# Strips of one weight group and back products of the group before it take turns, and the work behind a strip is spread over later chunks

## The chip, the cores and the metric

The kernel runs on one core of a Trainium2 chip. The metric is the device time of one execution in microseconds (us). Of the core's engines, TensorE (PE) does the matmuls, VectorE (DVE) and ScalarE (ACT) do the elementwise work that reads and writes the matmul accumulators (PSUM), GpSimd (POOL) prepares the weights, and SyncE (SP) issues the DMAs. Each engine works through its own list of instructions in order. They wait for one another through semaphores.

## The reference

Windowed attention with sinks for 2 batches x 8 heads x 768 positions x 64, then two feed-forward layers on the 1536 tokens (512 wide):

```python
keep = is_sink | in_window            # 4 sinks, window 128
a = softmax(where(keep, scale * q @ k.T, -1e9))
x = (a @ v) as 1536 x 512
# layer B, 1536 hidden columns
g = x @ w_gate
x = (g * sigmoid(g) * (x @ w_val)) @ w_out
# layer C, 2048 hidden columns
h = x @ w_in
out = (max(h, 0) + alpha * min(h, 0)) @ w_out2
```

## The kernel before

Every matmul operand is kept as a rounded part and the rest (`_hi`, `_lo`), and a product is three matmuls: hi x hi, hi x lo, lo x hi. A weight group g is 256 hidden columns: layer B has groups 0 to 5, of which group 5 comes first in what follows, layer C has groups 0 to 7. The tokens are three blocks of 512: block 0 ("single") is computed plainly, blocks 1 and 2 ("the pair") together, by a Strassen-like scheme.

The list `plan` sets the order of everything. Its entries for PE are chunks:

- a **front** (line 1881): a hidden tile of block 0, in two halves of 6 matmuls;
- a **strip** (line 1940): 6 matmuls, one of the 7 products (numbers 0 to 6) that together make one *set*, that is the four hidden tiles h11, h12, h21, h22 of the pair (first digit: half of the group, second: block 1 or 2). Layer B has two sets for a group, the gates set (in the banks of `att_ps`) and the values set (one bank of `att_ps`, two of `ffn_ps`), layer C one set;
- a **back product** (line 1966), here also "back": 6 matmuls, hidden tiles times output weights. A pair group has 8: four for block 1, which read h11 and h21, then four for block 2, which read h12 and h22.

What follows a strip: ACT copies strip 0 aside (`keep`, line 2098). DVE adds strips together in five `mix` steps 0 to 4, behind strips 1, 3, 4, 5, 6 (lines 2232, 2235, 2238, 2241, 2244). Strip 2 waits for `keep`, strips 3, 5 and 6 wait for mixes 0, 1 and 2. In layer B, ACT makes `silu` of the gates (line 2066). In layer C it makes `relu`, two instructions a tile (lines 2085, 2087). Then every hidden tile goes through three steps: **product** on DVE (2283 in B, 2294 in C), **rounding** on ACT (2108), **rest** on DVE (2300). In the plan, `("hidden", h)` stands for product and rounding, `("rest", h)` for the rest. The first of the back products of a block waits for the rests of both hidden tiles that it reads. A strip that starts in a bank waits until the tile that stood there is used up: the first strip in a bank of a layer C set waits for the rest of the tile of the set ahead, h11 for strip 0, h21 for strip 1, h12 for strip 4. Behind every back DVE takes the result out of PSUM (`evac`, 2309, 2325).

`emit(chunk, now, *later)` (line 888) writes the chunk, the events `now`, then what earlier chunks left for this place, and leaves `later[0]` for the next chunk, `later[1]` for the one behind it. Before the change layer B runs, group by group, 7 gates strips of group g+1, 8 backs of group g, 7 values strips of group g+1. Layer C runs 7 strips of group g+1, then 8 backs of group g. POOL prepares the weights in its own order (`jobs`), far ahead.

## Time and profile before

| | |
|---|---|
| median of 3 runs | 639.23 us (639.03 to 640.42) |
| the profiled execution | 640.56 us, its span 638.8 us |
| PE busy | 622.8 us, 97% of the span |
| DVE, ACT, POOL busy | 410.1, 244.3, 451.8 us (64%, 38%, 71%) |
| chain that ended last | PE 85%, DVE 7%, ACT 3%, issue 3% |
| granted clock of PE in every slice | 9 tenths or more |

To read it: a matmul instruction of 512 columns is shown as busy for about 0.39 us but the next one starts about 0.23 us later, so they overlap, and a busy PE can still start chunks late. What counts is the distance between the starts of chunks.

The strips begin at 227 us with those of layer B group 5. Layer B's pair runs until 421 us, with fronts between. Layer C's strips begin at 443 us, and its last matmul starts at 635 us.

### The profile page before, as it was taken

What the parts mean: (1) busy time and instruction counts of PE and PEld (TensorE: products, weight loads), DVE (VectorE), ACT (ScalarE), POOL (GpSimd) and SP (SyncE); (2) the same over time, 40 slices, a digit from 0 to 9 for tenths busy, and PEclk for the clock granted to TensorE, in tenths of its full rate; (3) what the DMA queues carried; (4) which work ended last, traced back from release to release, by engine and by line L of the source; (5) the groups of instructions that cost most, each with busy time, mean ns of one, the idle gap of its engine ahead of it and who ended that gap; (6) DMA issues with size and microseconds to landing.
All of it is one profiled execution on the core that took longest, in us unless ns stands there. A gap on an engine that the chain in (4) does not pass through costs nothing.

```text
span 638.8 us, 9474 instructions
## 1 busy us (share of the span) xinstructions
PE 622.8 (97%) x3072; PEld 488.0 (76%) x3072; DVE 410.1 (64%) x696; ACT 244.3 (38%) x585; POOL 451.8 (71%) x600
## 2 busy tenths in 40 slices
PE   8889999999999999999999999999999999999998
PEld 5467676776776888878788878888788888888886
DVE  4954566655476876564656474799686567756474
ACT  4735644545534642121212121435544333442150
POOL 6848698796985889998989664779999887810000
PEclk9999999999999999999999999999999999999999
DMA  9343323311331011221202222000212222000004
GB/s 299 110 149 110 123 80 136 117 51 50 100 95 43 30 35 34 76 74 48 67 33 67 82 84 63 25 30 16 67 67 66 67 66 84 17 0 1 1 14 184
DMA packets 29391, 45.67 MB, mean 71 GB/s; under 512 B 2880, under 2 KB 9024, under 8 KB 29344
## 3 DMA queue, kind: packets, MB, share of 16 engines
q1 hardware_dynamic: 29200, 44.81, 21.7%
q8 instruction: 25, 0.41, 0.3%
q10 hardware_dynamic: 144, 0.26, 0.1%
q14 instruction: 22, 0.18, 0.1%
HBM read 41.92 MB, written 3.15 MB: 71 GB/s over the span
## 4 chain that ended last, share of the span: by engine, by line
PE 85%; DVE 7%; ACT 3%; issue 3%; DMA 1%; POOL 0%; SPq 0%; DVEq 0%; ACTq 0%; POOLq 0%
PE ffn_ps L1966 27%; PE att_ps L1940 22%; PE ffn_ps L1881 14%; PE att_ps L1966 7%; PE ffn_ps L1940 6%; PE att_ps L1830 3%; PE att_ps L1792 2%; PE att_ps L1809 1%; DVE scratch L2193 1%; ACT scratch L2008 1%; PE att_ps L1881 1%; DVE scratch L2309 1%; ACT L2008 1%; DMA raw_weights<-pieces 1%; PE ffn_ps L1830 1%
## 5 line engine op out<-in xcount | busy, mean ns | idle before, releaser
L1653 POOL TENSOR_TENSOR w_lo<-raw_weights,w_hi 128x512 fp32r<-128x512 f32 (+1 forms) x128 | 154.4, 1206 | 10.3
L1652 POOL CAST w_hi<-raw_weights 128x512 fp32r<-128x512 f32 (+1 forms) x128 | 79.2, 619 | 38.0 <-PE ffn_ps L1966 20.5
L2309 DVE TENSOR_TENSOR scratch<-ffn_ps,scratch 128x512 f32<-128x512 f32 x112 | 76.4, 687 | 34.9 <-PE ffn_ps L1966 34.2
L1681 POOL TENSOR_TENSOR w_lo<-part_sum,w_hi 128x256 fp32r<-128x256 f32 x80 | 61.1, 764 | 6.4
L1881 PE MATMUL ffn_ps<-x_hi,w_hi 128*128 128x512 f32 x152 | 61.8, 406 | 2.1 <-DVE x_lo L2330 1.0
L1881 PE MATMUL ffn_ps<-x_hi,w_lo 128*128 128x512 f32 x152 | 59.5, 391 | 0.0
L1881 PE MATMUL ffn_ps<-x_lo,w_hi 128*128 128x512 f32 x152 | 59.2, 390 | 0.0
L1733 POOL TENSOR_TENSOR scratch<-scratch,inv 128x264 f32<-128x264 f32 (+1 forms) x48 | 31.2, 649 | 31.8 <-DVE inv L2182 31.5
L1966 PE MATMUL ffn_ps<-h_hi,w_hi 128*128 128x512 f32 x130 | 51.6, 397 | 0.0
L1966 PE MATMUL ffn_ps<-h_hi,w_lo 128*128 128x512 f32 x130 | 50.7, 390 | 0.0
L1966 PE MATMUL ffn_ps<-h_lo,w_hi 128*128 128x512 f32 x130 | 50.6, 389 | 0.0
L2098 ACT ACTIVATE value_sb<-att_ps 128x512 f32<-128x512 f32 x14 | 8.4, 600 | 100.3 <-PE att_ps L1940 100.3
L1940 PE MATMUL att_ps<-t_hi,w_hi 128*128 128x512 f32 x112 | 44.5, 398 | 1.3 <-DVE gate_sb L2232 0.8
L1940 PE MATMUL att_ps<-t_hi,w_lo 128*128 128x512 f32 x112 | 44.0, 392 | 0.0
L1940 PE MATMUL att_ps<-t_lo,w_hi 128*128 128x512 f32 x112 | 43.7, 391 | 0.0
L1940 PE MATMUL att_ps<-x_hi,w_hi 128*128 128x512 f32 x108 | 42.7, 395 | 0.0
L1940 PE MATMUL att_ps<-x_hi,w_lo 128*128 128x512 f32 x108 | 42.5, 393 | 0.0
L1940 PE MATMUL att_ps<-x_lo,w_hi 128*128 128x512 f32 x108 | 42.1, 390 | 0.0
L2003 ACT ACTIVATE bias<-top 128x2 f32<-128x2 f32 x48 | 9.8, 203 | 75.5 <-DVE top L2177 75.0
L1680 POOL CAST w_hi<-part_sum 128x256 fp32r<-128x256 f32 x80 | 34.7, 434 | 5.1
L2166 DVE COPY_PREDICATED att_ps<-take_prev,att_ps 128x256 f32<-128x256 int32 x34 | 14.4, 425 | 35.8 <-PE att_ps L1792 22.3
L2087 ACT ACTIVATE gate_sb<-gate_sb,minus_alpha 128x512 f32<-128x512 f32 x48 | 34.8, 725 | 1.6
(207 smaller groups left out, 1574.9 us busy)
## 6 DMA issues: line engine op xcount, KB each, us to landing
raw_weights<-pieces SPq DMA_DIRECT2D x122, 256.0 KB, 2.7
k_sb<-kt SPq DMA_DIRECT2D x12, 264.0 KB, 3.4
v_sb<-vt SPq DMA_DIRECT2D x12, 256.0 KB, 2.7
out<-scratch SPq DMA_DIRECT2D x12, 256.0 KB, 2.0
q_sb<-qt SPq DMA_DIRECT2D x11, 256.0 KB, 3.5
scratch<-vs SPq DMA_DIRECT2D x1, 384.0 KB, 5.5
q_sb<-qt ACTq DMA_DIRECT2D x1, 256.0 KB, 2.8
alpha<-alpha_t SPq DMA_DIRECT2D x1, 8.0 KB, 6.6
```

The source lines that it names most:

```text
L1652: chain(pool.tensor_copy(hi, raw[:, r % n_raw, at]))
L1653: last = pool.tensor_tensor(lo, raw[:, r % n_raw, at], hi.bitcast(F32), ALU.subtract)
L1680: chain(pool.tensor_copy(hi, s))
L1681: pool.tensor_tensor(lo, s, hi.bitcast(F32), ALU.subtract).then_inc(split_done, 1)
L1733: pool.tensor_tensor(rows, rows, inv[:, u % 4, :].unsqueeze(2).to_broadcast([P, 2, cols - at]), ALU.mult).then_inc(norm_done, 1)
L1830: last = pe.matmul(x[d, g, :], v_sb[:, ring, g, d], pt_sb[:, u % 2, m, h, :], start=g == 0 and m == 0, stop=not has_prev(c), skip_group_ch ...
L1881: last = pe.matmul(ps, w_parts[a][:, block_cols(kk)], x_parts(kk)[b], start=kk == 0 and (a, b) == (0, 0), stop=kk == n_k - 1 and (a, b) == ...
L1940: last = pe.matmul(ps, w_parts[a][:, block_cols(at * half_k + kk)], b_parts[b][:, kk, :], start=first and kk == 0 and (a, b) == (0, 0), st ...
L1966: last = pe.matmul(ps, lhs, rhs, start=f == 0 and (a, b) == (0, 0), stop=f == F - 1 and (a, b) == (1, 0))
L2087: act.activation(gate_of(h), gate_of(h), ACT.Copy, scale=minus_alpha[:, col:col + 1]).then_inc(relu_done, 1)
L2166: last = dve.copy_predicated(own_keys, take_prev[:, :].bitcast(mybir.dt.int32).unsqueeze(1).to_broadcast([P, 2, P]), s[:, :, 0:P])
L2309: ins = dve.tensor_tensor(total, back_ps(key), total, ALU.add)
```

## The change

The chunks stand in another order, by a new helper `weave`. In layer B the gates strips of group g+1 are put between the backs of group g for block 1: strips 0, 1, 2, back, 3, back, 4, back, 5, back, 6. The values strips are put between the backs for block 2: 0, back, 1, back, 2, back, 3, back, 4, 5, 6. For the first pair group (5) the gates strips take turns with the backs of layer C group 2, and its values strips stand alone. In layer C strips and backs alternate one by one: 0, back, 1, back, ..., 6, back, back. The first two sets of C are exceptions: group 0 runs 0, back, 1, 2, 3, back, 4, back, 5, 6, back, group 1 runs 0, 1, back, 2, back, ...

The events behind a strip move too. The backs of layer B for the pair use two banks of `ffn_ps` in turn, where they used five, and a wait of the values strips for an evac falls away. No instruction is added or dropped.

```diff
+    def weave(first, second, ahead):
+        order, left = [], list(first)
+        for n, chunk in zip(ahead, second):
+            order += left[:n] + [chunk]
+            left = left[n:]
+        return order + left
...
             elif g[0] == "B":
-                now = {2: [("hidden", h11)], 3: [mixes[1]], 4: [mixes[2], ("rest", h11), ("hidden", h22)],
-                       5: [mixes[3], ("hidden", h21)], 6: [mixes[4], ("rest", h22)]}[i]
-                emit(chunk, now, *([[("hidden", h12)], [("rest", h21)], [("rest", h12)]] if i == 6 else []))
+                now, later = {2: ([("hidden", h11)], [[], [], [("rest", h11)]]), 3: ([mixes[1]], []),
+                              4: ([mixes[2]], [[("hidden", h22)]]), 5: ([mixes[3]], [[("hidden", h21)]]),
+                              6: ([mixes[4]], [[("rest", h22), ("hidden", h12)], [("rest", h21)], [("rest", h12)]])}[i]
+                emit(chunk, now, *later)
             else:
-                now = {2: [("relu", h11)], 3: [mixes[1]], 4: [mixes[2], ("relu", h22), ("hidden", h11)],
-                       5: [mixes[3], ("relu", h21), ("rest", h11)], 6: [mixes[4], ("relu", h12), ("hidden", h22)]}[i]
-                emit(chunk, now, *([[("hidden", h21)], [("rest", h22)], [("hidden", h12)], [("rest", h21)], [("rest", h12)]]
-                                   if i == 6 else []))
+                now = {2: [], 3: [mixes[1]], 4: [mixes[2]], 5: [mixes[3]], 6: [mixes[4]]}[i]
+                done = {2: h11, 4: h22, 5: h21, 6: h12}.get(i)
+                if done:
+                    emit(chunk, now + [("relu", done)], [], [("hidden", done)], [("rest", done)])
+                else:
+                    emit(chunk, now)
...
-    fill = fronts(groups_c[1]) + backs(groups_c[0]) + fronts(groups_c[2]) + backs(groups_c[1]) + strips(pair_b[0], 0)
+    fill = (fronts(groups_c[1]) + backs(groups_c[0]) + fronts(groups_c[2]) + backs(groups_c[1])
+            + weave(strips(pair_b[0], 0), backs(groups_c[2]), (2, 1, 1, 1)))
...
+    plan_b = strips(pair_b[0], 1)
+    for g, ahead in zip(pair_b, pair_b[1:]):
+        in_gates, in_values = ([("back", (g, t, d)) for d in range(4)] for t in pair)
+        plan_b += weave(strips(ahead, 0), in_gates, (3, 1, 1, 1)) + weave(strips(ahead, 1), in_values, (1, 1, 1, 1))
...
-    turn = (backs(groups_c[3]) + fronts(groups_c[4]) + fronts(groups_c[5]) + backs(groups_c[4]) + strips(groups_c[0], 0))
+    turn = (backs(groups_c[3]) + fronts(groups_c[4]) + fronts(groups_c[5]) + backs(groups_c[4])
+            + weave(strips(groups_c[0], 0), backs(groups_c[5]), (1, 3, 1, 2)))
...
+    for g, ahead in zip(groups_c, groups_c[1:]):
+        plan_c += weave(strips(ahead, 0), pair_backs(g), (2 if g == groups_c[0] else 1,) + 6 * (1,) + (0,))
...
-                home = (rest_of_b if g != pair_b[-1] else (2, 3, 4, 0, 1, 2, 3, 4))[4 * (t - 1) + d]
+                home = d % 2 if g != pair_b[-1] else (2, 3, 4, 0, 1, 2, 3, 4)[4 * (t - 1) + d]
...
-                    if kind == "V":
-                        pe.wait_ge(evac_done, max(n for key, n in back_no.items() if back_home[key] == 2 + role and n < back_no[m[0], 1, 0]))
```

The order on DVE where a values set of layer B ends and the next gates set begins (lines 2232 to 2244 are the mixes, 2283 products, 2300 rests), before:

```order
L2300 TENSOR_TENSOR h_lo<-att_ps,h_hi 128x512
L2283 TENSOR_TENSOR value_sb<-value_sb,gate_sb 128x512
L2241 TENSOR_TENSOR ffn_ps<-ffn_ps,value_sb 128x512
L2283 TENSOR_TENSOR ffn_ps<-ffn_ps,gate_sb 128x512
L2244 TENSOR_TENSOR ffn_ps<-ffn_ps,value_sb 128x512
L2300 TENSOR_TENSOR h_lo<-value_sb,h_hi 128x512
L2283 TENSOR_TENSOR ffn_ps<-ffn_ps,gate_sb 128x512
L2232 TENSOR_TENSOR gate_sb<-att_ps,gate_sb 128x512
L2300 TENSOR_TENSOR h_lo<-ffn_ps,h_hi 128x512 x2
L2235 TENSOR_TENSOR gate_sb<-att_ps,gate_sb 128x512
```

The same place on DVE in the changed kernel, whose lines are numbered 4 higher:

```order
L2304 TENSOR_TENSOR h_lo<-att_ps,h_hi 128x512
L2242 TENSOR_TENSOR value_sb<-ffn_ps,value_sb 128x512
L2245 TENSOR_TENSOR ffn_ps<-ffn_ps,value_sb 128x512
L2287 TENSOR_TENSOR value_sb<-value_sb,gate_sb 128x512
L2248 TENSOR_TENSOR ffn_ps<-ffn_ps,value_sb 128x512
L2287 TENSOR_TENSOR ffn_ps<-ffn_ps,gate_sb 128x512
L2304 TENSOR_TENSOR h_lo<-value_sb,h_hi 128x512
L2287 TENSOR_TENSOR ffn_ps<-ffn_ps,gate_sb 128x512
L2236 TENSOR_TENSOR gate_sb<-att_ps,gate_sb 128x512
L2304 TENSOR_TENSOR h_lo<-ffn_ps,h_hi 128x512 x2
L2313 TENSOR_TENSOR scratch<-ffn_ps,scratch 128x512
```

The rest of h11 and the products of h22 and h21 changed places with mixes 2 to 4. From the rest of h22 on, the order is the old one, except that evacs now follow at once: the first back stands three strips behind the set, where it stood seven.

The order on DVE where the set of layer C group 0 ends and that of group 1 begins (2241, 2244 mixes 3 and 4, 2294 products, 2309 evacs), before:

```order
L2244 TENSOR_TENSOR att_ps<-att_ps,value_sb 128x512
L2294 SCALAR_TENSOR_TENSOR value_sb<-value_sb,gate_sb 128x512
L2309 TENSOR_TENSOR scratch<-att_ps,scratch 128x512
L2294 SCALAR_TENSOR_TENSOR att_ps<-att_ps,gate_sb 128x512
L2309 TENSOR_TENSOR scratch<-ffn_ps,scratch 128x512
L2300 TENSOR_TENSOR h_lo<-value_sb,h_hi 128x512
L2309 TENSOR_TENSOR scratch<-ffn_ps,scratch 128x512
L2294 SCALAR_TENSOR_TENSOR att_ps<-att_ps,gate_sb 128x512
L2309 TENSOR_TENSOR scratch<-att_ps,scratch 128x512
L2300 TENSOR_TENSOR w_lo<-att_ps,w_hi 128x512 x2
L2232 TENSOR_TENSOR value_sb<-att_ps,value_sb 128x512
```

The same place on DVE in the changed kernel:

```order
L2245 TENSOR_TENSOR att_ps<-att_ps,value_sb 128x512
L2298 SCALAR_TENSOR_TENSOR value_sb<-value_sb,gate_sb 128x512
L2248 TENSOR_TENSOR att_ps<-att_ps,value_sb 128x512
L2304 TENSOR_TENSOR h_lo<-value_sb,h_hi 128x512
L2313 TENSOR_TENSOR scratch<-att_ps,scratch 128x512
L2298 SCALAR_TENSOR_TENSOR att_ps<-att_ps,gate_sb 128x512
L2304 TENSOR_TENSOR w_lo<-att_ps,w_hi 128x512
L2298 SCALAR_TENSOR_TENSOR att_ps<-att_ps,gate_sb 128x512
L2236 TENSOR_TENSOR value_sb<-att_ps,value_sb 128x512
L2304 TENSOR_TENSOR w_lo<-att_ps,w_hi 128x512
```

Four evacs stood between mix 4 and the rest of h21. One is left, since only one back now stands between strip 6 of group 0 and strip 0 of group 1; and the rest of h22 now stands ahead of the product of h21.

## Rows read from the trace of the kernel before

**Rows 1.** Waits of PE, 227 to 640 us: us in total, times, longest.

```profile
PE att_ps L1940 <- DVE gate_sb L2232: 0.8, 2, 0.6
PE att_ps L1940 <- DVE w_lo L2300: 0.4, 1, 0.4
```

**Rows 2.** Chain of waits: start us, us, what, matmuls.

```profile
475.54 1.36 PE att_ps L1966 x6
...
479.62 9.66 PE att_ps L1940 x42
489.28 1.38 PE att_ps L1966 x6
```

**Rows 3.** Timeline of PE, last strips: start us, us, instruction, idle before and releaser.

```profile
312.60 0.40 PE L1940 MATMUL att_ps<-x_hi,w_hi 128*128 128x512 f32 x1
...
317.48 0.47 PE L1940 MATMUL att_ps<-t_hi,w_hi 128*128 128x512 f32 x1 [0.56 <-DVE gate_sb L2232]
317.79 0.40 PE L1940 MATMUL att_ps<-t_lo,w_hi 128*128 128x512 f32 x1
...
318.94 0.39 PE L1940 MATMUL att_ps<-t_hi,w_hi 128*128 128x512 f32 x1
```

**Rows 4.** Timeline of DVE, the same stretch.

```profile
311.24 1.02 DVE L2283 TENSOR_TENSOR value_sb<-value_sb,gate_sb 128x512 f32<-128x512 f32 x1
312.19 0.69 DVE L2241 TENSOR_TENSOR ffn_ps<-ffn_ps,value_sb 128x512 f32<-128x512 f32 x1
312.97 0.70 DVE L2283 TENSOR_TENSOR ffn_ps<-ffn_ps,gate_sb 128x512 f32<-128x512 f32 x1
313.58 0.69 DVE L2244 TENSOR_TENSOR ffn_ps<-ffn_ps,value_sb 128x512 f32<-128x512 f32 x1
314.18 1.72 DVE L2300 TENSOR_TENSOR h_lo<-value_sb,h_hi 128x512 fp32r<-128x512 f32 x1
315.82 0.69 DVE L2283 TENSOR_TENSOR ffn_ps<-ffn_ps,gate_sb 128x512 f32<-128x512 f32 x1
316.64 0.69 DVE L2232 TENSOR_TENSOR gate_sb<-att_ps,gate_sb 128x512 f32<-128x512 f32 x1
317.25 1.28 DVE L2300 TENSOR_TENSOR h_lo<-ffn_ps,h_hi 128x512 fp32r<-128x512 f32 x2
319.14 0.69 DVE L2235 TENSOR_TENSOR gate_sb<-att_ps,gate_sb 128x512 f32<-128x512 f32 x1 [0.61 <-PE att_ps L1940]
```

**Rows 5.** Timeline of PE at another start of a gates set.

```profile
343.64 0.40 PE L1940 MATMUL att_ps<-x_hi,w_hi 128*128 128x512 f32 x1
```

**Rows 6.** Timeline of DVE there.

```profile
347.54 0.68 DVE L2300 TENSOR_TENSOR h_lo<-ffn_ps,h_hi 128x512 fp32r<-128x512 f32 x1
```

**Rows 7.** DVE instructions on value_sb, 240 to 405 us: ns min/median/max.

```profile
L2283 DVE TENSOR_TENSOR value_sb<-value_sb,gate_sb x6: 680/1032/1422, 250.4 to 403.3; 128x512 f32<-128x512 f32 x6
...
L2300 DVE TENSOR_TENSOR h_lo<-value_sb,h_hi x5: 683/1028/1720, 253.0 to 375.9; 128x512 fp32r<-128x512 f32 x5
```

**Rows 8.** Timeline of ACT, the stretch of rows 4.

```profile
313.71 0.60 ACT L2108 ACTIVATE h_hi<-ffn_ps 128x512 fp32r<-128x512 f32 x1 [0.78 <-DVE ffn_ps L2283]
314.20 0.59 ACT L2098 ACTIVATE gate_sb<-att_ps 128x512 f32<-128x512 f32 x1
```

**Rows 9.** Timeline of PE, one strip of stage C.

```profile
460.19 0.47 PE L1940 MATMUL att_ps<-t_hi,w_hi 128*128 128x512 f32 x1 [0.39 <-DVE w_lo L2300]
```

**Rows 10.** Timeline of DVE, stage C.

```profile
530.39 0.69 DVE L2300 TENSOR_TENSOR w_lo<-att_ps,w_hi 128x512 fp32r<-128x512 f32 x1 [0.64 <-ACT w_hi L2108]
531.00 0.69 DVE L2244 TENSOR_TENSOR att_ps<-att_ps,value_sb 128x512 f32<-128x512 f32 x1
```

**Rows 11.** Timeline of ACT, the same stretch.

```profile
529.78 0.58 ACT L2108 ACTIVATE w_hi<-att_ps 128x512 fp32r<-128x512 f32 x1
...
531.80 0.60 ACT L2085 ACTIVATE gate_sb<-att_ps 128x512 f32<-128x512 f32 x1 [0.20 <-DVE att_ps L2244]
...
533.06 0.62 ACT L2108 ACTIVATE w_hi<-value_sb 128x512 fp32r<-128x512 f32 x1
```

More of the change, by code:

```diff
@@ L1010, in parts_of_sums @@
         return [(stage, name, kk) for name in T_PARTS for kk in range(half_k)]
-    fill = fronts(groups_c[1]) + backs(groups_c[0]) + fronts(groups_c[2]) + backs(groups_c[1]) + strips(pair_b[0], 0)
+    fill = (fronts(groups_c[1]) + backs(groups_c[0]) + fronts(groups_c[2]) + backs(groups_c[1])
+            + weave(strips(pair_b[0], 0), backs(groups_c[2]), (2, 1, 1, 1)))
     steps = parts_of_sums("B")
-    low_after = dict(zip((6, 8, 9, 10, 11, 14, 16, 18), steps))
+    low_after = dict(zip((6, 8, 9, 10, 11, 14, 16, 19), steps))
     high_after = dict(zip((5, 7, 8, 9, 10, 13, 15, 17), steps))
@@ L1022, in build_windowed @@
             plan.append(("thi", high_after[n]))
-    for n, g in enumerate(pair_b):
-        if n == 0:
-            for chunk in backs(groups_c[2]) + strips(g, 1):
-                emit_chunk(chunk)
-        if n + 1 < len(pair_b):
-            for chunk in strips(pair_b[n + 1], 0) + pair_backs(g) + strips(pair_b[n + 1], 1):
-                emit_chunk(chunk)
+    plan_b = strips(pair_b[0], 1)
+    for g, ahead in zip(pair_b, pair_b[1:]):
+        in_gates, in_values = ([("back", (g, t, d)) for d in range(4)] for t in pair)
+        plan_b += weave(strips(ahead, 0), in_gates, (3, 1, 1, 1)) + weave(strips(ahead, 1), in_values, (1, 1, 1, 1))
+    for chunk in plan_b:
+        emit_chunk(chunk)
     for chunk in fronts(groups_c[3]):
@@ L1054, in build_windowed @@
             plan.append(("thi", high_after[n]))
-    waiting = backs(groups_c[5])
-    for g in groups_c:
-        if g != groups_c[0]:
-            for chunk in strips(g, 0):
-                emit_chunk(chunk)
-        for chunk in waiting:
-            emit_chunk(chunk)
-        waiting = pair_backs(g)
+    plan_c = []
+    for g, ahead in zip(groups_c, groups_c[1:]):
+        plan_c += weave(strips(ahead, 0), pair_backs(g), (2 if g == groups_c[0] else 1,) + 6 * (1,) + (0,))
         if g[1] >= n_alone:
-            for chunk in fronts(g) + waiting:
-                emit_chunk(chunk)
-            waiting = backs(g)
-    for chunk in waiting:
+            plan_c += backs(g)
+        if ahead[1] >= n_alone:
+            plan_c += fronts(ahead)
+    for chunk in plan_c + pair_backs(groups_c[-1]) + backs(groups_c[-1]):
         emit_chunk(chunk)
@@ L1099, in build_windowed @@
     back_home, front_home, bank_ahead, had = {}, {}, {}, {}
-    rest_of_b = (2, 3, 4, 0, 1, 4, 0, 1)
     in_turn = (3, 4, 0, 1)
```

## The prediction

> **What bounds the kernel now.** I read the waits of the tensor engine first. From the first strip on, PE lost 0.8 us in two waits on a mix and 0.4 us in one wait on a rest [rows 1]. The chain of waits is one row of strips and back products after another: a back takes 1.36 us, seven strips 9.66 us, so 1.38 each, and the first back behind strips 1.38 [rows 2]. So the kernel is bound by the pace at which PE starts matmuls, and a new order can win only what PE still loses at waits. Read by starts, a wait is a little larger than the idle time shown. Take the start of a gates set of layer B, T = 312.60. Strip 3 should start 3 x 1.385 = 4.16 us later and starts at 317.48, 0.72 late. The matmul behind it follows after 0.31 us instead of 0.23, which adds 0.09 [rows 3]. Four gates sets have such a place, this is the largest, and all four come to about 1.9 us. Layer C has one, 0.39 us idle, about 0.5 by starts [rows 9]. More than 2.4 us of waits is not there to be won.
>
> The reason for 317.48 is DVE's list. Mix 0, on which strip 3 waits, stands behind the rest of h22 and the product of h12 and ends at 317.33. Strip 3 starts 0.15 later [rows 3, 4].
>
> **What the change removes.** In the gates sets a back now stands between strips 2 and 3, so strip 3 comes 1.36 us later, more than its lateness of 0.72. In the values sets and the other sets no strip waited before, and the same mixes now have a back of 1.36 us more. So the 1.9 us of layer B go. The dropped evac wait of the values strips showed no time: 0. The two banks for layer B's backs: evacs are done 0.9 us after a back's end (0.20 until DVE starts, as 318.94 to 319.14, and 0.69 [rows 3, 4]), and a bank now comes again two chunks later, 1.36 us at the least, so 0. If the evac were queued behind two more DVE operations, it would show. POOL's order of work is the old one but for two output pieces of layer C, and PE never waited for POOL in these stages [rows 1], so nothing there.
>
> **What it adds in layer B.** The first back of block 1 waits for the rest of h21. It stood seven strips behind T and now stands three behind it, at T + 4.15. When is that rest there? Before: the rest of h22 starts at T + 1.58, the product of h12 at T + 3.22, mix 0 at T + 4.04, the rest of h21 at T + 4.65. It takes 0.68 [rows 6], and PE follows 0.15 later: T + 5.48 [rows 3, 4]. In the new order these four stand in the same sequence. What stands ahead of them is turned round: mix 3 can start 0.20 after its strip, T - 1.18; then the product of h22 at T - 0.58, 0.95 to the next (311.24 to 312.19), mix 4 at T + 0.37, the product of h21 at T + 0.97, the rest of h22 at T + 1.57, with 0.60 for each step. That is the old 1.58. So the rows of before give the new times as they are: the back starts 5.48 - 4.15 = 1.33 us late at this place. At the best one, T = 343.64, the rest of h21 starts at 347.54, T + 3.90, and the lateness is 3.90 + 0.83 - 4.15 = 0.58 [rows 5, 6]. The two others lie between. I take the middle, 0.95, for four places. They differ by how long DVE needs for the two operations on value_sb, 0.68 to 1.72 us [rows 7]. At the fifth place, between groups 5 and 0, both are short (0.68), but the rest of h11 comes in behind mix 3 there, because no backs stand between the values strips: mix 3 at T - 1.18, then six steps of 0.60 up to the product of h12 at T + 2.4, mix 0 0.82 later (as 315.82 to 316.64), the rest of h21 0.61 later at T + 3.85, the back at 4.68: 0.5 late. With 0.09 behind each stop: 4 x 0.95 + 0.5 + 5 x 0.09 = 4.8 us. Bounds: with all operations at 0.68 the rest of h21 is bound by strip 1 (its end T + 2.77, mix 0 at 2.97, rest at 3.58, back at 4.41), 0.25 late at five places, 1.3 us; with 1.33 at each, 7.1 us. ACT lies in the same place: the product of h21 now ends at T + 1.67, was 1.07. Its rounding stands ahead of `keep` (313.71 and 314.20 before, T + 1.11 and 1.60 [rows 8]); `keep` shifts to about T + 2.2 and ends at T + 2.8, when strip 2 is to start (2.77). Some 0.1 us, and inside the lateness of the back, which is counted from T.
>
> On the two operations with value_sb: they took 680 ns at the least, 1.03 us in the median and up to 1.72 [rows 7], and the same instructions with one input in PSUM took 0.68 to 0.70 throughout [rows 4]. The Trainium skill, "SBUF — State Buffer", section "Who interferes with whom", says that a `tensor_tensor` with both inputs in SBUF contends with GpSimd for the shared port and that the loser blocks until the other has finished. By that rule the place of each stop would hang on where GpSimd happens to be, and a set could cost anything between the bounds above; by the rows as they fell, 0.95. The sum takes the rows.
>
> **What it adds in layer C.** First the place between groups 0 and 1. Strip 1 of group 1 starts in the bank of h21 of group 0 and waits for its rest. Between strip 5 of group 0, which completes h21, and this strip stand strip 6, one back and strip 0; there were strip 6, four backs and strip 0. Count from E, the end of strip 5. Mix 3 starts at E + 0.20. From a mix's start, `relu` begins 0.80 later, and the next ACT operation behind its two instructions 2.06 later (531.00, 531.80, 533.06) [rows 10, 11]. So the rounding of h22 is at E + 2.26 and ends at 2.88, its rest at 2.91, the evac of the back at 3.5, the product of h21 at 4.1, ready at 4.8, its rounding until 5.45, its rest 0.03 later (529.78 + 0.58 to 530.39) [rows 10, 11] until 6.2, PE at 6.3. Strip 1 would start at E + 1.38 + 1.36 + 1.38 = 4.1. It is 2.2 us late, 2.3 with the echo. Bounds: 1.5 (if evac and rest of h22 cost nothing) and 3.2 (if an operation on value_sb takes 1.7).
>
> Then the steady sets, groups 1 to 5, each followed by the first back of its block 1. From E: rest of h22 at 2.91, mix 4 behind it at 3.5 (though its strip ends at 2.74), `relu` of h12 from 4.3, and only behind that the rounding of h21, 3.5 + 2.06 = 5.6 to 6.2, its rest 6.2 to 6.9, PE at 7.0. The back stands five chunks behind E, 6.8. Late by 0.2 at five places: 1.0 us. Bounds: 0, and 0.7 each (3.5) where the rest of h22 takes 1.0 more. Before, these rests had four to seven chunks more, and no wait.
>
> **The pace.** Chunks behind a strip take 1.38 to 1.39, others 1.36 [rows 2]. The number of chunks that follow a strip is the same in any order, but more of them are now backs: -0.3 us. Bounds 0 and -2.5 (every strip at 1.36).
>
> **The sum.** -1.9 + 4.8 - 0.5 + 2.3 + 1.0 - 0.3 = +5.4 us. On the profiled execution, 640.56 us (span 638.8 and 1.8 around it), that is 646.0. The median of the runs is 639.23, 1.3 lower, so I forecast 644.5 for it. What a measurement of this kernel tells from no change is 0.2%, 1.3 us.
>
> **Rivals.** (1) *Faster.* The rests are there in time, because DVE, relieved of the crowd behind strips 4 to 6, is earlier than I count. Then the old waits go and no new one comes: -1.9 - 0.5 - 0.3, 636.5 us. It decides at one point: the rest of h21 would have to end by T + 4.0 instead of 4.6 to 5.3, and strip 1 of layer C's group 1 to find its rest 2.2 us earlier. For it: DVE is idle for a third of the time. Against it: mix 0 can't start before strip 1 has ended, so even the lower bound is 0.25 late. (2) *The waits come out at their lower bounds* in layer B (1.3) and in the steady sets (0), and only the place between groups 0 and 1 stands: -1.9 + 1.3 - 0.5 + 2.3 - 0.3 = +0.9, 640.1 us. For it: the operations on value_sb are short when GpSimd is idle, and the steady sets' 0.2 is the difference of two long sums. Against: GpSimd works through most of both layers. (3) *The pace wins more.* Every strip behind a back runs at 1.36: about -2 instead of -0.3, 642.8 us. For it: the first strip behind backs does. Against: the first back behind strips runs at 1.38, so the slow chunk may only have moved. (4) *Worse*: value_sb's operations long at each place, and the steady sets late by 0.5: 4.8 becomes 6.5 and 1.0 becomes 2.5, 647.7 us.
>
> **How the numbers follow.** The forecast 0.50, (1) 0.08, (2) 0.14, (3) 0.13, (4) 0.15. The range 640.4 to 647.4 leaves out (1), part of (2) and half of (4). Faster by over 0.2%: (1) and a tail of (2), 0.10. Within 0.2%, 638.0 to 640.5: half of (2) and little else, 0.10. Slower: 0.80.
>
> **What would show it.** In the profile after: PE idle before the first back of block 1 behind strip 2 of a gates set, with the rest (line 2304) as releaser, 0.5 to 1.3 us at five places; about 2 us before strip 1 of layer C's group 1, near 460 us, with the same releaser; small stops on the same kind of back in layer C's later sets; and no more wait of strip 3 on mix 0. If the first of these is missing, my count of DVE's list is wrong. If strips and backs that alternate all keep 1.36, the pace term is.

## The result, and the profile after

| | before | after |
|---|---|---|
| median | 639.62 us (639.03 to 640.42, 4 runs) | 651.39 us (650.87 to 651.84, 4 runs) |
| ratio | 1 | 1.0184, 95% interval 1.0171 to 1.0196 |
| profiled execution, its span | 640.56, 638.8 us | 651.24, 649.5 us |
| start of the first strip to start of the last matmul | 408.2 us | 418.7 us |

The change costs 11.8 us between the medians and 10.7 us between the two profiled executions. Both profiles start their strips at 227 us, so 10.5 us of it lie between there and the last matmul. The waits of PE from the first strip on, in the changed kernel (total, times, longest; before: [rows 1]):

```profile
PE ffn_ps L1970 <- DVE h_lo L2304: 2.6, 5, 0.6
PE att_ps L1944 <- DVE w_lo L2304: 2.4, 1, 2.4
PE ffn_ps L1970 <- DVE w_lo L2304: 1.1, 1, 1.1
PE att_ps L1970 <- issue: 0.3, 1, 0.3
PE att_ps L1944 <- ACT gate_sb L2102: 0.2, 1, 0.2
```

The waits of strip 3 on mix 0 are gone. Five first backs wait for a rest in layer B (line 1970), one strip waits 2.4 us in layer C, and one first back waits 1.1 us there. That is 6.6 us of idle time against 1.2 before, 5.4 of the 10.5 us.

A wait's idle time is not the whole price, because an engine that is late by less than 0.1 to 0.3 us shows no idle row. So I took the start of every chunk in both traces and subtracted 1.36 us for each, the fastest that a chunk ever ran ([rows 2] has it for backs):

| excess over 1.36 us per chunk | before | after |
|---|---|---|
| stops in layer B, with the chunk behind | 1.9 | 5.8 |
| stop between groups 0 and 1 of layer C, with the chunk behind | 0.65 | 2.7 |
| stops in layer C's steady sets | 0 | 2.7 |
| stops at fronts and at the turn to layer C | 0.35 | 0.6 |
| slow chunks without a stop | 3.0 | 4.6 |
| sum | 5.9 | 16.4 |

A stop is a chunk that starts late because PE waited.

The chain of waits in the changed kernel at the boundary between two groups, with T = 346.32 as the start of strip 0 of the next gates set (start us, us, what):

```profile
342.34 2.77 PE ffn_ps L1944 x12
345.13 0.04 DVE ffn_ps L2245
...
345.74 0.82 DVE value_sb L2287
...
346.86 0.69 DVE ffn_ps L2248
347.55 0.13 DVE ffn_ps L2287
...
348.06 1.27 DVE h_lo L2304
349.33 0.62 DVE ffn_ps L2287
...
350.07 0.57 DVE gate_sb L2236
...
350.68 0.69 DVE h_lo L2304
351.37 0.24 issue
351.62 1.62 PE ffn_ps L1970 x6
353.24 1.39 PE att_ps L1944 x6
354.63 1.39 PE ffn_ps L1970 x6
```

From 345.13 to 351.37 no PE row is in the chain. The end of the kernel hangs on DVE's list: mix 3, product of h22, mix 4, product of h21, rest of h22, product of h12, mix 0, rest of h21. PE's first back starts at 351.62, T + 5.30. With no wait it would start at T + 4.15, the place that the prediction counted for it. Two DVE instructions stand out, the product of h22 (1.20 us) and the rest of h22 (1.27 us). Both have only SBUF inputs. Beside them stand GpSimd's rows:

```profile
344.41 0.61 POOL L1658 CAST w_hi<-raw_weights 128x512 fp32r<-128x512 f32 x1
345.10 1.29 POOL L1659 TENSOR_TENSOR w_lo<-raw_weights,w_hi 128x512 fp32r<-128x512 f32 x1
346.33 1.07 POOL L1658 CAST w_hi<-raw_weights 128x512 fp32r<-128x512 f32 x1
347.49 1.29 POOL L1659 TENSOR_TENSOR w_lo<-raw_weights,w_hi 128x512 fp32r<-128x512 f32 x1
348.72 0.86 POOL L1658 CAST w_hi<-raw_weights 128x256 fp32r<-128x256 f32 x1
```

DVE's product is issued at 345.74. GpSimd's subtraction ends at 346.39, and the product 0.55 later. DVE's rest is issued at 348.06, the next subtraction ends at 348.78, and the rest again 0.55 later. Each lasts as long as GpSimd's instruction still ran, and then 0.55. GpSimd's conversion at 346.33 was issued behind the product and lasts 1.07 us, where the same instruction took 0.61 at 344.41. So each waits for the one that came first.

### The profile page after: what moved, and what is told of

It is laid out like the page before. It is cut to its first block, busy times and chain, and to the rows that moved or that the text cites. A ratio compares the mean times of both kernels' runs of the same rounds, so it can differ in the third digit from the quotient of the medians.

```text
span 649.5 us, 9454 instructions
## 1 busy us (share of the span) xinstructions
PE 627.1 (97%) x3072; PEld 487.1 (75%) x3072; DVE 414.1 (64%) x696; ACT 244.6 (38%) x585; POOL 454.3 (70%) x600
## 4 chain that ended last, share of the span: by engine, by line
PE 82%; DVE 9%; ACT 4%; issue 4%; DMA 1%; POOL 0%; SPq 0%; DVEq 0%; ACTq 0%; POOLq 0%
PE ffn_ps L1970 28%; PE att_ps L1944 19%; PE ffn_ps L1887 13%; PE att_ps L1970 6%; PE ffn_ps L1944 6%; PE att_ps L1836 2%; PE att_ps L1798 2%; DVE h_lo L2304 2%; PE att_ps L1815 1%; DVE scratch L2197 1%; ACT scratch L2012 1%; PE att_ps L1887 1%; ACT L2012 1%; DMA raw_weights<-pieces 1%; PE ffn_ps L1836 1%
## 5 line engine op out<-in xcount | busy, mean ns | idle before, releaser
L1658 POOL CAST w_hi<-raw_weights 128x512 fp32r<-128x512 f32 (+1 forms) x128 | 82.9, 648 | 45.5 <-PE att_ps L1944 18.8
L2313 DVE TENSOR_TENSOR scratch<-ffn_ps,scratch 128x512 f32<-128x512 f32 x116 | 79.1, 687 | 53.9 <-PE ffn_ps L1970 52.9
L1970 PE MATMUL ffn_ps<-h_hi,w_hi 128*128 128x512 f32 x140 | 56.3, 402 | 2.6 <-DVE h_lo L2304 2.6
L1970 PE MATMUL ffn_ps<-h_hi,w_lo 128*128 128x512 f32 x140 | 54.9, 392 | 0.0
L1970 PE MATMUL ffn_ps<-h_lo,w_hi 128*128 128x512 f32 x140 | 54.6, 390 | 0.0
L2089 ACT ACTIVATE gate_sb<-att_ps 128x512 f32<-128x512 f32 x26 | 15.5, 597 | 53.6 <-PE att_ps L1944 31.3
```

The lines of the kernel that those rows point to most:

```text
L1658: chain(pool.tensor_copy(hi, raw[:, r % n_raw, at]))
L1970: last = pe.matmul(ps, lhs, rhs, start=f == 0 and (a, b) == (0, 0), stop=f == F - 1 and (a, b) == (1, 0))
L2089: act.activation(gate_of(h), front_of(h, 0), ACT.Relu, scale=-1.0).then_inc(relu_done, 1)
L2313: ins = dve.tensor_tensor(total, back_ps(key), total, ALU.add)
```

## The experiments

`before` was measured again beside them. Its medians were 639.31 us beside the first four experiments, 639.76 beside the next four (up to "The old order with the rests moved"), 640.47 beside T tiles that hold x, T tiles elsewhere and the turns from strip 5, and 640.36 beside the two with T tiles low. Ratios are to these.

**The change in layer B alone.** Plan, events and banks of layer C as before.

Against the changed kernel, in part:

```diff
-                now = {2: [], 3: [mixes[1]], 4: [mixes[2]], 5: [mixes[3]], 6: [mixes[4]]}[i]
...
+                now = {2: [("relu", h11)], 3: [mixes[1]], 4: [mixes[2], ("relu", h22), ("hidden", h11)],
...
-            + weave(strips(groups_c[0], 0), backs(groups_c[5]), (1, 3, 1, 2)))
...
-        plan_c += weave(strips(ahead, 0), pair_backs(g), (2 if g == groups_c[0] else 1,) + 6 * (1,) + (0,))
...
+        if g != groups_c[0]:
+            for chunk in strips(g, 0):
+                emit_chunk(chunk)
+        for chunk in waiting:
+            emit_chunk(chunk)
```

> The changed kernel with layer C put back: order of chunks and events of layer C as before, layer B (and the backs of layer C group 2 among its first gates set) as changed. The theory 'waits on rests and on keep, plus a slower pace' adds up from the two traces, by starts of chunks: layer B lost 1.9 us at stops before and 5.8 after, and 1.7 then 2.4 us by slower chunks, so +4.6 us against the kernel before, 644.2. The rival 'one place decides, the 2.6 us stop in layer C' says that layer B alone is within 2 us of the kernel before.

Measured: 645.51 us, ratio 1.0096 (1.0081 to 1.0111), +6.2 us. The stops in layer B, by starts, are those of the full change to 0.02 us: 5.8 us. The sum of the excess is 10.8.

**The change in layer C alone.**

Layer B keeps its order, events and banks of before. Against the kernel before, in part:

```diff
-                now = {2: [("relu", h11)], 3: [mixes[1]], 4: [mixes[2], ("relu", h22), ("hidden", h11)],
...
+                    emit(chunk, now + [("relu", done)], [], [("hidden", done)], [("rest", done)])
...
+            + weave(strips(groups_c[0], 0), backs(groups_c[5]), (1, 3, 1, 2)))
...
+        plan_c += weave(strips(ahead, 0), pair_backs(g), (2 if g == groups_c[0] else 1,) + 6 * (1,) + (0,))
```

> The changed kernel with layer B put back, layer C as changed. By the same sums layer C lost 0.7 us at stops before and 5.6 after, and 1.3 then 2.2 us by slower chunks: +5.9 us against the kernel before, 645.5. If the two layers act on each other (later use of the PSUM banks, POOL's place in time), the two parts don't add up to the 10.5 us between the two traces; by the theory they do, within 1 us.

Measured: 645.96 us, 1.0101 (1.0083 to 1.0118), +6.65 us. By the medians the two halves give 6.2 + 6.65 = 12.85 us against 11.8, and by starts 4.9 + 5.2 = 10.0 against 10.5. The second sum comes that near in part by luck. Three things differ in this execution. Its 5.2 us hold 1.6 us in which TensorE's granted clock had fallen to half (shown under "Strips 1, 3, 4 and 5 read x"), and the changed kernel's profiled execution has none of that. Layer B stopped for 1.0 us less than in the profile of before. And the wait of 1.1 us in layer C is not there: the stop in that place costs 0.4 us in place of 1.4. With all three set right the two halves give 4.9 + 5.6 = 10.5. This run also showed what layer B's order of before costs in another execution. Its stops came to 0.84 us there, not 1.88. The one of 0.72 us from which the prediction was read [rows 3] was 0.07. DVE, ACT and GpSimd work through the same lists in both runs up to there. What differs is the rest of h22. Before it took 1.72 us [rows 4]. Here:

```profile
313.86 1.03 DVE L2306 TENSOR_TENSOR h_lo<-value_sb,h_hi 128x512 fp32r<-128x512 f32 x1
```

**The first C set whole, four backs between it and the next.**

```diff
-    turn = (backs(groups_c[3]) + fronts(groups_c[4]) + fronts(groups_c[5]) + backs(groups_c[4])
-            + weave(strips(groups_c[0], 0), backs(groups_c[5]), (1, 3, 1, 2)))
+    turn = (backs(groups_c[3]) + fronts(groups_c[4]) + fronts(groups_c[5]) + backs(groups_c[4]) + strips(groups_c[0], 0)
+            + backs(groups_c[5]))
```

> The changed kernel, but the first set of layer C runs as before: seven strips, then the four backs of group 5. So four backs stand between strip 6 of group 0 and strip 0 of group 1. Theory 'strip 1 of group 1 waits for the rest of h21 of group 0': the stop of 2.6 us near 463 us goes, and the first set has fewer slow chunks: 2.7 us less than the changed kernel. Rival 'DVE and ACT are simply behind at this place': the stop moves to the first back of group 0 or to a later strip, and less than 1.3 us is won.

Measured: 647.14 us, 1.0121 (1.0105 to 1.0136), 4.0 us less than the full change by the ratios. The wait of 2.4 us is gone, 2.7 us with the chunk behind, as expected. The one of 1.1, which was at the first back of group 2, is gone too, and the sets there stop for 0.3 to 0.4 us each. That 1.0 us isn't owed to this edit: the runs that keep the first C set as changed (layer C alone, old events in B, short subtractions) stop for 0.3 us at this back as well.

**The events alone, with the old order of chunks.**

Against the kernel before, in part; `weave` isn't used and the banks are those of before:

```diff
-                now = {2: [("hidden", h11)], 3: [mixes[1]], 4: [mixes[2], ("rest", h11), ("hidden", h22)],
...
+                now, later = {2: ([("hidden", h11)], [[], [], [("rest", h11)]]), 3: ([mixes[1]], []),
...
-                now = {2: [("relu", h11)], 3: [mixes[1]], 4: [mixes[2], ("relu", h22), ("hidden", h11)],
...
+                    emit(chunk, now + [("relu", done)], [], [("hidden", done)], [("rest", done)])
```

> The old order of chunks in both layers, with the new places of the events. Nothing of layer C should stop now, since the backs again stand behind the strips: -0.6. In layer B the rest of h11 comes behind mix 3 in each values set, because no backs stand between the strips, so the product of h22 and all behind it, mix 0 too, come 0.6 us later than before: strip 3 about 1.0 us late at five places where it was 0.5 at four. Theory: +2.5 us against the kernel before and no slower pace. Rival 'the new events are what costs': +5 us or more. Rival 'the taking of turns alone costs': within 1.3 us.

Measured: 647.67 us, 1.013 (1.0115 to 1.0145), +8.4 us. I had expected 2.5. Its waits:

```profile
PE att_ps L1951 <- ACT gate_sb L2109: 3.0, 5, 1.3
PE ffn_ps L1977 <- DVE scratch L2320: 1.0, 4, 0.3
```

The product of h21 stands behind mix 4 in the new events, its rounding stands ahead of `keep` on ACT, and strip 2 waits for `keep`: 0.4 to 1.5 us at each of the five boundaries. In layer C the evacs come late, and the backs wait for their banks. The spread of the events is no relief by itself. It puts work that nobody needs yet ahead of work that PE waits for. The new order of layer C with its old events was not tried.

**The new order with layer B's old events.**

```diff
-                now, later = {2: ([("hidden", h11)], [[], [], [("rest", h11)]]), 3: ([mixes[1]], []),
...
+                now = {2: [("hidden", h11)], 3: [mixes[1]], 4: [mixes[2], ("rest", h11), ("hidden", h22)],
+                       5: [mixes[3], ("hidden", h21)], 6: [mixes[4], ("rest", h22)]}[i]
...
```

> The changed kernel with its order of strips and backs, but in layer B the hidden state's steps stand where they stood before (product of h22 right behind strip 4, rest of h11 with it, product of h21 behind strip 5, rest of h22 behind strip 6, then the product of h12, the rest of h21). My theory: DVE has one step less between mix 3 and the product of h12 (the product of h22 and the rest of h11 are done before mix 3), so the rest of h21 comes about 0.5 us earlier and the rounding of h21 no longer delays `keep`. The five boundary sets of layer B then stop 0.3 to 0.5 us each in place of 1.2: 5.8 becomes about 2.5, 3.3 us less than the changed kernel, 648.1 us. Rival: the stops are set by the order of chunks alone (first back of block 1 three strips behind the set in place of seven) and by the lengths of the value_sb operations: no change, 651.4.

Measured: 651.41 us, 1.0177 (1.0163 to 1.019), no change. Layer B's stops come to 6.0 us by starts, 5.8 in the changed kernel. The stops of strip 2 on `keep` (0.35 to 0.43) go, as I expected, and the first back is late by 1.0 to 1.2 in place of 0.6 to 0.85. The step that DVE saves is lost in the rest of h22, which takes 1.72 us in place of 1.27:

```profile
347.42 1.72 DVE L2303 TENSOR_TENSOR h_lo<-value_sb,h_hi 128x512 fp32r<-128x512 f32 x1
```

**GpSimd's subtractions cut short.**

The low parts of the other columns are left out. One of the two places of the edit:

```diff
+                if late_now:
+                    at, hi, lo = slice(at.start, at.start + 64), hi[:, 0:64], lo[:, 0:64]
                 last = pool.tensor_tensor(lo, raw[:, r % n_raw, at], hi.bitcast(F32), ALU.subtract)
```

> The changed kernel, but from the start of the strips on GpSimd's subtractions that make the low parts of the weights (1.29 us for 128x512, 0.73 for 128x256) cover 64 columns only; the low parts of the other columns are left out. DVE's, ACT's and PE's instructions are the same. My theory: DVE's operations with both inputs in SBUF (the product and the rest of h22, on value_sb) last 1.0 to 1.7 us in place of 0.68 because they wait until a subtraction on GpSimd has ended, and that sets how long the stops are. Then they fall to about 0.7, layer B's stops from 5.8 to about 1.8 us (0.25 and the echo at five places), the stop at layer C's groups 0 and 1 from 2.6 to about 1.5, the later ones from 2.7 to under 0.5: 7 us less, about 644.3. Rival: their length has another cause (other accesses to SBUF): no change, 651.4. Rival 2: DVE's length falls but the stops hang on the dependencies alone: 650.

Measured: 647.26 us, 1.0118 (1.0104 to 1.0131), 4.2 us less than the full change. The operations on `value_sb` in layer B, changed kernel and then this one (min, median and max in ns):

```profile
L2287 DVE TENSOR_TENSOR value_sb<-value_sb,gate_sb x6: 685/1196/1198, 252.1 to 409.0; 128x512 f32<-128x512 f32 x6
...
L2304 DVE TENSOR_TENSOR h_lo<-value_sb,h_hi x5: 1061/1271/1272, 253.9 to 379.7; 128x512 fp32r<-128x512 f32 x5
```

```profile
L2293 DVE TENSOR_TENSOR value_sb<-value_sb,gate_sb x6: 681/682/837, 251.8 to 405.7; 128x512 f32<-128x512 f32 x6
...
L2310 DVE TENSOR_TENSOR h_lo<-value_sb,h_hi x6: 678/724/805, 253.6 to 407.7; 128x512 fp32r<-128x512 f32 x6
```

They fall to their shortest, and the first backs of layer B stop for 0.25 to 0.38 us: 5.8 us became 2.7. The mechanism is shown. The size that I expected, 7 us, was not reached, because layer C gained little: 2.2 between groups 0 and 1 in place of 2.6, and in the steady sets the stops of 0.3 to 0.4 stay. Those hang on the order and not on GpSimd: the operations on `value_sb` are at 0.68 us there in any case. This profile also holds 1.6 us at a granted clock of 0.50 behind the long wait, which the profile of the changed kernel has not.

**Strips 1, 3, 4 and 5 read x instead of T.** Now the pace. These strips compute with other inputs than they should.

```diff
-                b_parts = operands[b_name]
+                b_parts = operands[{"T1": "B11", "T2": "B21", "T3": "B11", "T4": "B21"}.get(b_name, b_name)]
```

> The changed kernel, but strips 1, 3, 4 and 5 read tiles of x as their moving operand (B11, B21, B11, B21) in place of T1 to T4; the T tiles are still made, and the products of these strips are those of other inputs. Theory one: a strip is slow (1.384 to 1.390 us against 1.360) because of the T tile that it reads, and so is the chunk behind it. Then all strips and backs run at 1.360: the 4.6 us that the chunks lie above 1.360 without a stop fall to under 0.5, 647.0 us. Theory two: the slow chunks come from the strip's place behind another chunk, from its weights or from its waits: the pace stays 1.384 and the time 651.4.

Measured: 648.53 us, 1.014 (1.0125 to 1.0156). Layer C in the chain of waits, changed kernel and then this one:

```profile
538.36 1.39 PE att_ps L1944 x6
539.75 1.39 PE ffn_ps L1970 x6
541.14 1.39 PE att_ps L1944 x6
542.52 1.39 PE ffn_ps L1970 x6
```

```profile
538.78 1.36 PE att_ps L1944 x6
540.14 1.36 PE ffn_ps L1970 x6
541.50 1.36 PE att_ps L1944 x6
542.86 1.36 PE att_ps L1970 x6
```

The 4.6 us of slow chunks are 0.1. In layers B and C a strip that reads a T tile is slow, and so is the chunk behind it, be it a strip or a back; the one behind that takes 1.381, and the next is back at 1.360. The time fell by 2.9 us and not by 4.5. That isn't owed to the stops: by starts they come to 11.7 us here and to 11.8 in the changed kernel. What takes back 1.6 us is TensorE's clock. Behind the wait between groups 0 and 1 of layer C, 2.64 us here, the granted clock fell to 0.50, which is the lower of its two levels, 1.2 GHz. The matmuls then start 0.43 us apart in place of 0.23 (timeline of PE, then one stretch with its granted clock in the third column from the right):

```profile
467.06 0.63 PE L1970 MATMUL ffn_ps<-w_lo,h_hi 128*128 128x512 f32 x1
467.49 0.63 PE L1970 MATMUL ffn_ps<-w_hi,h_lo 128*128 128x512 f32 x1
...
470.57 0.39 PE L1944 MATMUL att_ps<-x_lo,w_hi 128*128 128x512 f32 x1
```

```profile
467.00:470.00 3.00, 3.00 (x8) 2.34 (x7) 1.75 (x3) 0.00 (x0) 2.84 (x5) 0.50 0.33 90
```

The two chunks in this stretch take 1.14 and 0.47 us more than 1.36. The profiles of layer C alone, of the old events in B and of the short subtractions have the same stretch behind the same wait, at 461.65, 466.96 and 464.90 us, and lose 1.6 us by it. The profile of the changed kernel waits 2.44 us there and keeps its clock, but two of its four timed executions show a mean granted clock of 0.997, as these profiles do, where the others show 1.000. So the long wait can cost 1.6 us more than its own length. The run with the first C set whole, which has no such wait, shows 0.999 or more in all four executions.

**The old order with the rests moved.** The first stop that the prediction describes has a cheap remedy without a new order of chunks:

```diff
-                       5: [mixes[3], ("hidden", h21)], 6: [mixes[4], ("rest", h22)]}[i]
-                emit(chunk, now, *([[("hidden", h12)], [("rest", h21)], [("rest", h12)]] if i == 6 else []))
+                       5: [mixes[3], ("hidden", h21)], 6: [mixes[4]]}[i]
+                emit(chunk, now, *([[("hidden", h12)], [("rest", h22), ("rest", h21)], [("rest", h12)]] if i == 6 else []))
...
-                emit(chunk, now, *([[("hidden", h21)], [("rest", h22)], [("hidden", h12)], [("rest", h21)], [("rest", h12)]]
+                emit(chunk, now, *([[("hidden", h21)], [("rest", h22), ("rest", h21)], [("hidden", h12)], [("rest", h12)]]
```

> The kernel before with its order of strips and backs, and only the rests moved: in layer B the rest of h22 stands no longer right behind strip 6 but with the rest of h21, two chunks behind, so that mix 0 of the next set isn't behind it; in layer C the rest of h21 comes with the rest of h22, two chunks behind strip 6 in place of four. My theory: the stops of strip 3 on mix 0 in layer B (0.8 to 1.9 us) and that at layer C's groups 0 and 1 (0.65) go: 1.5 us faster than before, 637.8. Rival: the rest of h21, now behind the rest of h22, or the rest of h22 itself delays mix 1 and strip 5 in their turn, 0.3 us at each of five places: 639.3, as before.

Measured: 638.36 us, 0.9979 (0.9969 to 0.9989), 1.4 us faster than before. The view of PE's waits is empty from 227 us on (by starts 0.4 us are left at the fronts); mix 0 comes ahead of the rest of h22:

```profile
315.16 0.69 DVE L2232 TENSOR_TENSOR gate_sb<-att_ps,gate_sb 128x512 f32<-128x512 f32 x1 [0.43 <-PE att_ps L1940]
315.77 0.82 DVE L2300 TENSOR_TENSOR h_lo<-value_sb,h_hi 128x512 fp32r<-128x512 f32 x1
```

DVE is idle ahead of mix 0, so it starts as soon as strip 1 has ended. In [rows 4] the rest of h22 held up the product of h12, and that mix 0.

**What in a T tile is slow.** The next four stand on the 638.36 us kernel. First GpSimd copies a quarter of x into each T, so the strips with T compute with other values.

```diff
-                pool.tensor_tensor(sum_sb(stage, n)[at], a, b, ALU.subtract).then_inc(tsum_done, 1)
+                pool.tensor_copy(sum_sb(stage, n)[at], a).then_inc(tsum_done, 1)
```

> The kernel before with the rests moved (638.36 us, all of the tensor engine's waits behind the first strip gone but one), and GpSimd copies one of the two quarters of x into each T in place of their difference: the T tiles lie where they lay and hold values of x; the strips with T compute with those. Of the time, 3.2 us are chunks of 1.384 to 1.390 in place of 1.360, all of them strips that read a T tile or the chunk behind one. Theory one: it is what the tiles hold that slows the strip: the pace returns to 1.360, 635.2 us. Theory two: it is where the tiles lie, or that they are other tensors than x: 638.4, and the spacing stays.

Measured: 638.07 us, 0.9964 (0.9951 to 0.9977), and every strip at the old 1.373 to 1.390. The values aren't it.

Then T1 to T3 lie elsewhere:

```diff
+        value_sb = sb("value_sb", [P, 4, TB])
+        t_lo = sb("t_lo", [P, 3, half_k, TB], F32R)
         t_hi = sb("t_hi", [P, 3, half_k, TB], F32R)
-        t_lo = sb("t_lo", [P, 3, half_k, TB], F32R)
-        value_sb = sb("value_sb", [P, 4, TB])
```

> The same kernel (638.36 us) with the real T, but the memory of T1, T2 and T3 moved: value_sb comes first, then the low parts, then the high parts, so that every one of these tiles lies at another address; T4 stays. Theory one (the values set the pace): nothing changes, 638.4 us, strips 1, 3, 4 and 5 at 1.384 to 1.390. Theory two (the place in memory): strips 1, 3 and 4 and the chunk behind them change to 1.360, strip 5 with T4 stays slow, 636.2 us.

Measured: 638.62 us, 0.9972 (0.9962 to 0.9981), every strip as it was. But this moved the high parts up by 20 KB and the low parts down by 4 KB, all within the upper end of the partition. Then T4 alone went to the lower end:

```diff
+        with nc.sbuf_tensor("x2_sb", [P, n_k, TB], F32) as x2_sb:
+            pass
+        t4_hi = sb("t4_hi", [P, half_k, TB], F32R)
+        t4_lo = sb("t4_lo", [P, half_k, TB], F32R)
+
         raw = sb("raw_weights", [P, n_raw, PIECE])
...
```

> The 638.36 us kernel (the one before with the rests moved), and the tiles of T4 lie at the start of SBUF's partitions (byte 1152 to 9344) in place of 184768 to 192960; all other tensors below the attention block lie 8 KB higher, T1 to T3 where they were. Up to now every moving operand of a fast chunk (x, hidden state) lay below byte 146560 and every T tile above 184768. Theory one: a moving operand high up in the partition is what makes a chunk slow; then strip 5, which reads T4, runs at 1.360 in place of 1.373, and strip 6 behind it at some 1.381 in place of 1.389; 0.3 us in all, 638.0 us, and the spacing of strip 5 is what tells. Theory two: the place doesn't matter; strip 5 stays at 1.373 and strip 6 at 1.389.

Measured: 638.15 us, 0.9972 (0.996 to 0.9983), which can't be told from 638.36. The starts can. In ns, mean over all sets of layer B (without stops):

| | strip 4 | strip 5 (T4) | strip 6 | chunk behind |
|---|---|---|---|---|
| T4 high | 1373 | 1373 | 1389 | 1381 |
| T4 low | 1373 | 1389 | 1381 | 1360 |

I had expected strip 5 at 1360. It runs as a chunk with x does behind a T strip, 1389, and the two behind it are one step further on the way to 1360 (1381, then 1360). So T4 has become a fast operand, and theory one holds, but not with the number that I gave for strip 5.

**All T tiles low.** The attention block, T and `value_sb` come first, raw weights, `gate_sb` and the sums last. PE's moving operands now lie at bytes 1152 to 33920 (T) and 120192 to 177536 (x, hidden state); before, T began at 184768.

> The 638.36 us kernel with SBUF laid out anew: T4, the attention block and in its place T1 to T3 and value_sb come first (byte 1152 to 42112), then the weights, x and the hidden state (up to 177536), and the raw weights, gate_sb and the sums behind them. Order and instructions are the same. Theory one (moving operands above about 180 KB are slow): all strips and backs at 1.360, 3.2 us less, 635.2 us. Theory two (the place doesn't matter): 638.4. Theory three: what matters isn't T's tiles but any operand above byte 146560; then the strips with x low parts and the backs, now up to 177536, become slow too and the T strips fast: 640 us or more.

Measured: 636.12 us, 0.9939 (0.9927 to 0.9952), 4.2 us faster than before and 2.6 us faster than the kernel with T high by the ratios. The chain of waits, seven strips of layer C, was [rows 2]'s 9.66 us:

```profile
538.45 9.52 PE att_ps L1941 x42
547.97 1.36 PE att_ps L1967 x6
```

9.52 is seven times 1.36. The slow chunks fell from 3.2 us to 0.1. Some stops came back in layer B (0.9 us, the largest 0.34 on `keep`), since strips are faster now and ACT and DVE are not. This version beats both kernels. Between 177536 and 184768 lies a border for moving operands; which byte it is and why was not tried.

**Taking turns, but later.** Last, whether turns themselves cost. Layer C and the rests are those of the 638.36 us kernel. In layer B, against the changed kernel:

```diff
-        plan_b += weave(strips(ahead, 0), in_gates, (3, 1, 1, 1)) + weave(strips(ahead, 1), in_values, (1, 1, 1, 1))
+        plan_b += weave(strips(ahead, 0), in_gates, (5, 1, 1, 0)) + weave(strips(ahead, 1), in_values, (1, 1, 1, 1))
```

> The 638.36 us kernel, but in layer B strips and backs take turns as in the changed kernel, with one difference: in a gates set the first back of block 1 stands behind strip 4 in place of strip 2 (weave (5, 1, 1, 0)); layer C as before, the rests as in the 638.36 us kernel. My theory: the 5.8 us of stops that the changed kernel has in layer B are the first back standing too near behind the set: two strips later its rest is there (T + 5.6 against T + 6.9), no stop is left, and only the pace costs, 0.6 us for the backs that are slow behind a strip with T: 639.0 us. Rival: taking turns itself makes DVE late (an evac between the mixes of each strip), stops of 0.3 us or more at five or more places come back: 640.5 us or more.

Measured: 638.52 us, 0.9971 (0.9959 to 0.9983). Not one stop in layer B, where the changed kernel has 5.8 us. By starts it is 0.5 us longer than the 638.36 us kernel: 0.65 us more in slow chunks, the backs behind T strips, and 0.1 less in stops. So taking turns costs the pace alone, and the 5.8 us go with the first back's place, three strips behind the set, or with the place of the rests. The rests stand in the order of the 638.36 us kernel here, which is another difference from the changed kernel; how much of the 5.8 us that alone would win, with the back where it was, was not tried. The old events alone won nothing there (651.41 us).

## Why the prediction was wrong

The direction and the places were right. The forecast was +5.4, and +11.8 came (+10.5 by starts). The step that failed is the pace, which had the wrong sign; the stops had the right cause and were sized too small. By its own terms:

| term | predicted | measured |
|---|---|---|
| old stops of layer B go | -1.9 | -1.9 in this profile, -0.8 in another execution |
| new stops of layer B | +4.8 | +5.8 |
| old stop of layer C goes | -0.5 | -0.65 |
| strip 1 of group 1 waits | +2.3 | +2.7 |
| steady sets of C | +1.0 | +2.7 in this profile, +1.7 in four other executions |
| pace | -0.3 | +1.6 |
| fronts | 0 | +0.25 |

1. **The pace had the wrong sign.** "The number of chunks that follow a strip is the same in any order, but more of them are now backs" took slowness as something that a strip gives to its successor once, and less to a back. The runs show that it belongs to strips with T and to the chunk behind each. In the old order most of these are themselves strips with T; in the new one each T strip has a back of its own to slow down. [Rows 2] had only the mean, 9.66 us for seven strips. The starts of single strips would have shown 1.373 between two T strips and 1.389 behind them. This is 1.9 us of the error. The rival "the pace wins more" had the sign wrong too.
2. **The steady sets of layer C** were sized as the difference of two long sums, 7.0 - 6.8. Of the five first backs that of group 1 came in time. Those of groups 3 to 5 came 0.3 to 0.4 late and the chunk behind 0.1, which makes 0.4 to 0.5 a place in place of 0.2. At the back of group 2 the product of h22 took 1.42 us and its rest 1.69, and the back was late by 1.3. The bound that I gave for a place, 0.7, took one long operation, and there were two. That is 1.7 us. Of it 1.0 is chance of this execution: in the profiles of layer C alone, the first C set whole, the old events in B and the short subtractions the same back is 0.3 late, and the sets come to 1.7 us. Between groups 0 and 1 the rest of h22 took 1.10 us, which is the 0.4 there.
3. **The middle between two places was not the middle.** For layer B I took 0.95 between 0.58 and 1.33. The order of DVE's list came as counted: with T = 346.32, mix 3 at T - 1.19 and the product of h22 at T - 0.58, both as forecast, the rest of h22 at T + 1.74 (forecast 1.57) and the rest of h21 at T + 4.36 (4.65 and 3.90 at the two places of before). But over 1.36 us a chunk the lateness was 0.35 at strip 2 and 0.85 at the back at three of four places, 1.2 in all (1.15 by the 1.385 that the prediction took for a strip), 0.68 at the fourth, and 1.06 at the fifth where I had 0.5. Both operations on `value_sb` were long at the same spot of each of the three sets (products at 314.13, 345.74 and 377.37 us, 1.20 each), since GpSimd's subtraction started 0.64 us ahead of each. The prediction named the two instructions and said why they vary. The Trainium skill, "SBUF — State Buffer", section "Who interferes with whom", says that the second to issue blocks until the first has finished. The rows at 345.74 and 346.33 agree in both directions, and so does the run with short subtractions (1196 and 1271 ns down to 682 and 724). What failed is the use made of it: a middle value. Rows of GpSimd beside those of DVE tell why a place was long or short. How the two would meet in the changed kernel they could not tell, so the upper bound should have had more weight.
4. **`keep` was counted as hidden.** It was: the back's lateness is counted from T and holds it. But `keep` is why strip 2 is late by 0.35 us at three places, where the forecast had 0.1.
5. **The base.** The stop of 0.72 us at 317.48 was a long rest of h22 in one execution. The term of -1.9 was right for that profile, and 1 us too much for the execution with layer C alone. The profiled execution of before was 0.9 us above its median, which is most of the way from 10.7 to 11.8.

Of what was to show it: the first back's wait at five places came (0.4 to 0.6 us idle, 0.6 to 0.85 by starts), the 2.4 us near 460 us came at 467.45, and strip 3 waits no more. The sentence "if strips and backs that alternate all keep 1.36, the pace term is [wrong]" looked in one direction only.

## What to carry to other kernels

Before two streams are woven, count for each consumer how many chunks stand between it and the chain that feeds it, on the engine that runs the chain: a back moved from seven strips behind a set to three came 0.7 to 1.2 us late, and at five, with the rests later, it came in time. Put what PE waits for next ahead of what is only due later; steps spread evenly did the opposite. And read durations of a wide range row by row beside the other engine's rows before a middle is taken.

## What was not expected of the hardware

- A matmul whose moving operand lies at byte 184768 of the partition or above makes six matmuls take 1.373 to 1.390 us in place of 1.360, and so does the chunk behind. Up to byte 177536 it doesn't. The stationary operand was low in all runs, so nothing is known of it. It is worth 2.6 us of 638 here, for a new order of allocations.
- The same list of instructions differs by 1 us in one layer from execution to execution, as GpSimd and DVE meet at another point: the rest of h22 took 1.72 us in one and 1.03 in the other at the same place of layer B, and the first back of group 2 in layer C was 1.3 us late in one and 0.3 to 0.4 in five others.
- Behind a wait of 2.0 to 2.6 us TensorE's granted clock fell to 0.50 in four profiles and stayed at 1.00 in one, and the fall cost 1.6 us. Two of ten executions of the kernel with T4 low, whose profile has no such wait, show the mean clock of 0.997 too, at 640.15 and 640.57 us where the median is 638.15. They have no profile, so where the clock fell there isn't known.
